# Which expert block uses the third buffer for its second weight matrix, in a fused attention, MLP and expert kernel

## The reference

```python
x = attention(q, k, v)                   # window of 64 keys, 4 x 576 tokens, 8 heads of 64
h = x @ w_in                             # 2304 x 512 times 512 x 2048
x = (h * tanh(softplus(h))) @ w_out      # 2048 x 512
do_compute = x @ w_skip > 0              # other tokens leave as they are
e_idx = argmax(x @ w_gate)               # one of 8 experts
for e in range(8):
    h = maximum(x[mask] @ w1[e], 0)      # w1: 512 x 1024
    y[mask] = gate_w * (h @ w2[e])       # w2: 1024 x 512
out = x + y
```

## Time and profile before

| | |
|---|---|
| three runs | 710.62, 712.65, 714.82 us (median 712.65) |
| the profiled execution | 713.13 us, of it span 711.5 us |
| TensorE (PE) busy | 682.2 us (96%), 4958 matmuls |
| VectorE, ScalarE, GpSimd busy | 488.1, 357.4, 254.2 us |
| mean granted TensorE clock | 0.989 |
| expert blocks | 12, the last 11 from 552.1 us on |

### The profile page before, as it was taken

One profiled execution on the slowest core, in us unless ns is written; L12 is line 12 of the kernel. 1 busy time (PEld: TensorE's weight loads), 2 busy tenths in 40 slices (PEclk: granted clock), 3 DMA queues, 4 the chain that ended last, 5 costly groups with the idle time before them and its releaser, 6 DMA issues. The chain is left out here.

```text
span 711.5 us, 13645 instructions
## 1 busy us (share of the span) xinstructions
PE 682.2 (96%) x4958; PEld 604.0 (85%) x4958; DVE 488.1 (69%) x940; ACT 357.4 (50%) x784; POOL 254.2 (36%) x231
## 2 busy tenths in 40 slices
PE   6898999999999999999999999999999979999995
PEld 5776898879898989888989888987988969899894
DVE  5797767867776885785786686679589545455352
ACT  5555566555554565456545555453554053443350
POOL 4312342443352343353344344335553331221221
PEclk9899999999999999999999999999999999999998
DMA  9734131151244132125115114102647799999940
GB/s 275 236 101 141 46 98 38 38 98 44 69 91 104 50 78 82 39 63 109 38 38 134 39 37 99 38 1 60 237 140 262 228 392 354 346 345 357 342 176 2
DMA packets 62835, 97.16 MB, mean 137 GB/s; under 512 B 23015, under 2 KB 27111, under 8 KB 62769
## 3 DMA queue, kind: packets, MB, share of 16 engines
q1 hardware_dynamic: 59152, 91.01, 42.0%
q0 software_dynamic: 3168, 4.51, 2.1%
q10 hardware_dynamic: 448, 0.79, 0.4%
HBM read 84.97 MB, written 13.73 MB: 139 GB/s over the span
## 5 line engine op out<-in xcount | busy, mean ns | idle before, releaser
L1552 POOL TENSOR_TENSOR q_sb<-n_sb,r_sb 128x512 f32<-128x512 f32 x72 | 94.3, 1309 | 287.1 <-DVE a_sb L1141 163.0
L628 PE MATMUL Y<-wout_hi,g_hi 128*128 128x512 f32 x272 | 111.6, 410 | 3.2 <-ACT g_hi L885 3.0
L609 PE MATMUL H<-x_hi,win_hi 128*128 128x256 f32 x384 | 112.4, 293 | 2.0 <-DVE x_lo L1075 1.9
L609 PE MATMUL H<-x_hi,win_lo 128*128 128x256 f32 x384 | 108.9, 284 | 0.0
L609 PE MATMUL H<-x_lo,win_hi 128*128 128x256 f32 x384 | 108.8, 283 | 0.0
L628 PE MATMUL Y<-wout_lo,g_hi 128*128 128x512 f32 x272 | 107.3, 395 | 0.0
L1558 POOL TENSOR_TENSOR g_lo<-g_sb,g_hi 128x512 fp32r<-128x512 f32 x68 | 88.2, 1297 | 2.5 <-ACT g_hi L885 1.9
L721 PEld LDWEIGHTS H<-xT,w 128*128 128x128 f32 x768 | 87.6, 192 | 1.0
L721 PE MATMUL H<-xT,w 128*128 128x128 f32 x768 | 88.0, 275 | 0.0
L1121 DVE TENSOR_SCALAR u_sb<-e_sb 128x512 f32<-128x512 f32 x72 | 34.0, 472 | 73.8 <-ACT e_sb L870 73.0
L885 ACT CAST g_hi<-g_sb 128x512 fp32r<-128x512 f32 x68 | 42.2, 620 | 74.6 <-DVE g_sb L1154 72.4
(11 more groups left out here) (205 smaller groups left out, 1408.0 us busy)
## 6 DMA issues: line engine op xcount, KB each, us to landing
w<-moe_w SPq DMA_DIRECT2D x23, 2048.0 KB, 10.9
kT<-k_T SPq DMA_DIRECT2D x32, 256.0 KB, 3.0
vw<-v_w SPq DMA_DIRECT2D x32, 256.0 KB, 3.0
y_rows<-ytile SPq DMA_DIRECT2D x36, 128.2 KB
out_rows<-ytile SPq DMA_DIRECT2D x36, 128.0 KB
win<-moe_w_in SPq DMA_DIRECT2D x8, 512.0 KB, 8.5
qbd<-q_T SPq DMA_DIRECT2D x64, 64.0 KB, 2.6
wout<-moe_w_out SPq DMA_DIRECT2D x8, 512.0 KB, 7.9
```

The lines of the kernel that those rows point to most:

```text
L609: last = nc.tensor.matmul(HM3[J % 3][:, f, :], wt[:, j, d, f * P:(f + 1) * P], xt[:, c % 2, d, :], start=(n == 0), stop=(n == 3 * DB - 1))
L628: last = nc.tensor.matmul(Y[t][:, :], gt[:, J % 2, lo:lo + P], wt[:, 2 * j + f, :], start=(j == 0 and f == 0 and wt is wout_hi and gt is g ...
L1552: nc.gpsimd.tensor_tensor(q_sb[:, :], n_sb[:, J % 2, :], r_sb[:, J % 2, :], ALU.mult).then_inc(q_ok, 1)
```

## The change

Three things change.

- `w2t` holds the `w2` of block 3 (`spare(b)`: b is `EARLY`, which is 3) in place of block 2's. It is allocated ahead of `ot`, so that it shares memory with slices 0 to 3 of `wout_hi`. SP loads it in the last chunk, right behind block 1's `w1`, once slice 3 of the last chunk is multiplied down. Block 2's `w2` goes into buffer 0, when block 0's `expert_down` is done and block 2's rows are gathered. The load of block 3's `w2` after block 1 is gone.
- Block 3's expert is fixed with the second pick: `lowest_left` now has six dependent steps and runs in tick 0 of the last chunk; `pick_third` leaves that expert out as well.
- GpSimd waits for the placed tokens of chunk c - 2 in tick 1 of chunk c, in place of those of c - 1 in tick 7. For chunk 7's tokens the wait stays in tick 7 of the last chunk.

```diff
             with ExitStack() as raw:
                 w2 = sb("w2", [P, 2, EFB * D], FP32, raw)
             w2_lo = sb("w2_lo", [P, 2, EFB * D], F32R, exp_)
+            with ExitStack() as raw:
+                w2t = sb("w2t", [P, EFB * D], FP32, raw)
+            w2t_lo = sb("w2t_lo", [P, EFB * D], F32R, exp_)
             ot = sb("ot", [P, 2, D], FP32, exp_)
...
-        LSTEPS = 4
+        LSTEPS = 6
...
-        def third(b):
-            return isinstance(b, int) and b == 2
+        def spare(b):
+            return isinstance(b, int) and b == EARLY
...
         def w2_there(eng, b, bh, slot_):
-            if third(b):
+            if spare(b):
                 eng.wait_ge(w2t_in, 16)
-            elif slot_ % 2 == 0 and not (isinstance(b, int) and b == 0):
-                eng.wait_ge(w2_in[0], loaded(bh, slot_) - 16)
+            elif slot_ % 2 == 1 and not (isinstance(b, int) and b == 1):
+                eng.wait_ge(w2_in[1], loaded(bh, slot_) - 16)
...
                     sp.wait_ge(g1_ok, NJ * NC)
                     load_w2(es[1], 1)
                     load_w1(es[1], 1)
+                    sp.wait_ge(lowest, LSTEPS)
+                    e4 = early_expert(EARLY)
+                    sp.wait_ge(g2_ok, NJ * c + 4)
+                    load_w2t(e4)
                 if c > 0:
                     store_rows(c - 1)
...
             store_rows(NC - 1)
-            sp.wait_ge(g2_ok, NJ * NC)
+            sp.wait_ge(bz_ok, 1)
             sp.wait_ge(xs_in[2], 16)
-            load_w2t(e3)
-            sp.wait_ge(lowest, LSTEPS)
-            e4 = early_expert(EARLY)
+            load_w2(e3, 0)
             sp.wait_ge(bh_ok, 4)
             load_w1(e4, 1)
-            sp.wait_ge(bz_ok, 2)
-            load_w2(e4, 1)
             sp.wait_ge(tstep, TSTEPS)
...
             def pick_second():
...
+                lowest_left()
...
                 step, count = steps(lowest, 0)
-                atmax = df[:, 1, :]
-                step(nc.vector.tensor_tensor(atmax, early[:, :], rev[:, 0, :], ALU.mult))
+                shut, atmax = first[:, 0, :], df[:, 1, :]
+                step(nc.vector.tensor_scalar(shut, early[:, :], -1.0, 1.0, ALU.mult, ALU.add))
+                step(nc.vector.tensor_tensor(atmax, shut, rev[:, 0, :], ALU.mult))
                 step(nc.vector.reduce_max(turn[:, 0:1], atmax, AX.X))
+                step(nc.vector.scalar_tensor_tensor(out=shut, in0=rev[:, 0, :], scalar=turn[:, 0:1], in1=early[:, :],
+                                                    op0=ALU.is_equal, op1=ALU.add))
...
             nc.vector.tensor_copy(q_sb[:, :], PTB[:, :]).then_inc(yT1_ok, 1)
-            lowest_left()
             rest_of_w2(1, 1, 2)
...
                 if c > 0 and j == 6:
                     scatter_tokens(c - 1)
-                if c > 0 and j == 7:
+                if c > 1 and j == 1:
+                    all_placed(c - 2)
+                if c == NC - 1 and j == 7:
                     all_placed(c - 1)
```

More of the change, by code:

```diff
@@ L185, in build @@
             cbi_i = sb("cbi_i", [P, NV], I32, exp_)
-            with ExitStack() as raw:
-                w2t = sb("w2t", [P, EFB * D], FP32, raw)
-            w2t_lo = sb("w2t_lo", [P, EFB * D], F32R, exp_)
         with ExitStack() as exp_:
@@ L328, in blocks @@
                         block_of(i * RING + n, i, n)
-        def third(b):
-            return isinstance(b, int) and b == 2
+        def spare(b):
+            return isinstance(b, int) and b == EARLY
         def w2_raw(b, slot_):
-            return w2t[:, :] if third(b) else w2[:, slot_ % 2, :]
+            return w2t[:, :] if spare(b) else w2[:, slot_ % 2, :]
         def w2_rest(b, slot_):
-            return w2t_lo[:, :] if third(b) else w2_lo[:, slot_ % 2, :]
+            return w2t_lo[:, :] if spare(b) else w2_lo[:, slot_ % 2, :]
         def w2_there(eng, b, bh, slot_):
-            if third(b):
+            if spare(b):
                 eng.wait_ge(w2t_in, 16)
-            elif slot_ % 2 == 0 and not (isinstance(b, int) and b == 0):
-                eng.wait_ge(w2_in[0], loaded(bh, slot_) - 16)
+            elif slot_ % 2 == 1 and not (isinstance(b, int) and b == 1):
+                eng.wait_ge(w2_in[1], loaded(bh, slot_) - 16)
             else:
@@ L804, in expert_block @@
                     expert_up(b, bh, slot_, half)
-                mid = EFB // 2 if third(b) else 0
+                mid = EFB // 2 if isinstance(b, int) and b == 2 else 0
                 if mid:
@@ L1258, in pick_third @@
                 step(nc.vector.tensor_tensor(now, nextrow[:, :], ecap[:, :], ALU.subtract))
-                step(nc.vector.scalar_tensor_tensor(out=held, in0=early[:, :], scalar=-float(BIG), in1=now,
+                step(nc.vector.scalar_tensor_tensor(out=held, in0=first[:, 0, :], scalar=-float(BIG), in1=now,
                                                     op0=ALU.mult, op1=ALU.add))
```

## The result

| | before | after |
|---|---|---|
| median of 20 runs each | 711.70 us | 714.27 us |
| lowest and highest | 708.97 to 714.82 | 712.18 to 716.69 |
| ratio after to before | | 1.0041, 95% interval 1.0027 to 1.0054 |
| the profiled execution | 713.13, span 711.5 | 712.60, span 711.0 |

The change makes the kernel 2.6 us slower. The forecast summed its terms to +0.1, at 712.8; measured are +2.6. (The medians differ by 2.6. Of that, 2.3 us are in the first 70 us, which the change doesn't touch (the same transposes start at 67.97 and at 65.71). So what follows compares intervals inside a profile, and uses further profiles of both kinds.

What follows compares the result with a forecast made beforehand. The prediction took TensorE to set the time. Its terms, -1.3 + 0.9 + 0.5 + 0 = +0.1 us, gave 713.2 on the profiled execution, forecast as 712.8 against the median of 712.65, with a range of 709.5 to 717.0.

Steps and rivals of the forecast that it cites:

- GpSimd's wait in tick 1: Chunk 1: without the scatter wait in tick 7, TensorE's 1.31 us wait for `g_lo` goes: -1.3, bounds -1.3 and 0.
- The pick in tick 0: Last chunk: six VectorE steps ahead of `g_hi` make TensorE wait +0.9 us near 500, bounds 0 and +1.1.
- the rival's mechanism: Last chunk's pick: a GpSimd operation holds one of VectorE's new steps, adding 2.6 us, 715.4; chance 0.03.
- Block 2's `w2`: Load issued at 559.4 as before, arriving no sooner without block 3's load behind it: 0, bound -1.5; stall of 3.92 us stays.
- The faster rival: Block 2's matrix comes sooner without block 3's load, and its stall could go: -5.7, 707.0; chance 0.13.
- The load in the last chunk: `w2t` loaded behind block 1's matrices: 2.1 MB, 5.2 us of all DMA engines, cost 0 on SP's queues.
- GpSimd's small DMAs under that load: Chunk 7's scatter +2.6 us, block 2's gather -1.6; middle taken, +0.5, counted in full.
- the prediction's own sign of being wrong: TensorE waits before block 2's rows' transpose, rows land after 561, or block 2's stall differs by over 1 us.
- The half that was to come back: Block 2's gather, once SP's transfers are over, takes at most 3.1 us against 4.7: -1.6.
- The slower rival: The third load pushes block 2's rows back by the whole 5.2 us: +4.8, 717.5; chance 0.19.
- the clock behind the stall: Behind block 2's stall TensorE runs 2.8 us at 1.2 GHz, losing about 1.4 us; said to stay.
- The bounds: Whole kernel: the terms' bounds add up to -3.5 (-1.3 + 0.9 - 1.6 - 1.5) and +3.7 (0 + 1.1 + 2.6).

Runs made afterwards that it cites:

- e1: The kernel before with only GpSimd's wait for chunk c - 2's tokens moved to tick 1 (last chunk keeps tick 7): 710.25 us, ratio 0.9973.
- e3: The changed kernel with GpSimd's wait put back into tick 7 of every chunk: 715.13 us, ratio 1.0045.
- e2: The kernel before with only the fourth expert's pick moved to tick 0 of the last chunk, in six steps: 711.92 us, ratio 1.0003.
- e11: e7 with gathers issued ahead of the wait for output rows, and the fourth expert's six steps in tick 2 of the last chunk: 708.48 us, ratio 0.9929.
- e4: The changed kernel again, unaltered, for a second profile and more runs: 714.49 us, ratio 1.0034.
- e5: The changed kernel with the load of block 3's `w2` moved ahead of block 1's matrices, near 517: 711.63 us, ratio 0.9976.
- e7: The changed kernel with e5's edit and without SP's wait for block 2's rows ahead of block 2's `w2`: 712.63 us, ratio 0.9987.
- e8: e1's kernel without SP's wait for block 2's rows, so `w2t` is issued near 552: 710.94 us, ratio 0.9967.

## Why the prediction was right or wrong

**GpSimd's wait in tick 1: right.** Forecast -1.3; the wait of 1.31 is gone, and e1 alone gives -1.9 with an interval from about -3.6 to -0.1. The size was read from one execution: the waits of 0.6 and 0.2 us in e3 and e2 make the mean of three profiles 0.7.

**The pick in tick 0: right.** Forecast a wait of 0.9 for `g_hi` near 500; it is 0.79 at 498. In tick 0 GpSimd held none of the steps, as the order of operations had it; e11 shows that the rival's mechanism is real one tick further on.

**Block 2's `w2`: right.** Its time from issue to cast is 10.6 us against 10.8, and over the seven profiles 10.1 to 11.3 (after, e3, e4, e5) against 10.7 to 11.7 (before, e1, e2); block 3's load behind it had not held it up. Block 3's first cast waits for no DMA. The faster rival fails with it: the load wasn't slow because of what was removed.

**The load in the last chunk: right in its place, wrong in its size.** The prediction's term for "GpSimd's small DMAs under that load" is the one that was mis-sized. It put +0.5, the middle between -1.6 and +2.6. The seven profiles give +2.7, just above the upper bound, and the prediction's own sign of being wrong came: TensorE waits before the transpose of block 2's rows. In the means, 1.0 of the 2.7 fall between the scatter and the load of token numbers, for which the term had up to +2.6. The load of token numbers, which it put at nothing, takes 1.6 more up to the gather. The half that was to come back, a quicker gather once SP's transfers are over, didn't: from the gather's issue to that of block 2's `w2` are 5.1 to 5.6 us with the load (558.98 - 553.72 in e4) and 4.6 to 5.9 without, 0.2 more in the mean and not 1.6 less. The row taken for it, block 1's gather in an otherwise quiet stretch, resembled nothing behind block 2's token numbers, where `w1` and the output rows are moved in both kernels. The slower rival had the mechanism with half its price: 2.7 us fall on the line of rows 7 where it put 5.2. That the idle engines took up the rest, as the prediction argued against it, fits but isn't shown. The routed rows of chunk 7 were put near 547 and landed at 548.95, which is 551.6 in the time of the profile before; that cost nothing.

**Missed: the clock behind the stall.** The forecast kept 2.8 us of slow clock. The two profiles of the changed kernel have 6.0 and 4.9, for stalls of 3.8 and 4.0; e1, with a stall of 2.3, has none. e3 has 3.4 us of it behind its wait for the rows. The lines of e4 and e1:

```profile
576.20:581.10 4.90, 4.85 (x12) 3.82 (x13) 0.50 (x1) 0.00 (x0) 1.14 (x2) 0.50 0.90 367
```

```profile
572.90:575.70 2.80, 2.78 (x12) 2.31 (x13) 0.47 (x1) 0.00 (x0) 0.00 (x0) 1.00 1.05 402
```

The first is e4's, the second e1's, both over the first half of block 2's `expert_down`. The other runs suggest that these profiles happened to be slow for long. The mean granted clock of the whole kernel is 0.985 in both, and 0.9876 over the 32 runs of the changed kernel beside 0.9880 over the 35 of the kernel before on e4's chip. That is 0.3 us of slow clock more for the change, uncertain by about 1 us either way. It covers the whole kernel, so the stretch behind the stall isn't told by it alone.

**The sum again**, with the terms of the profiles: -1.3 + 0.8 + 2.7 = +2.2 against +2.6 measured. The 2.7 is TensorE's, from block 1's transpose to block 4's, and has the slow clock in it. Two terms are uncertain by about 1 us: the first is -0.7 by the mean of three profiles, and the clock's share of 1.2 in the 2.7 is larger than all the runs together have. That the sum comes so near is in part luck.

**The bounds.** The lower one, -3.5, was summed with +0.9 for the pick, whose own lower bound is 0; it should have been -4.4. The measured +2.6 is inside either way, but the range of 709.5 to 717.0 holds the base of 712.65 too, and so left the direction open.

**The base.** The median of three runs, 712.65, stood 0.95 above that of twenty; the 1.5 between 712.8 and 714.27 looks small by luck, for the change itself was missed by 2.5.

## What to carry to other kernels

Idle DMA engines aren't free if a line of small dependent transfers runs through them: here 2 MB in the gap before it delayed the end of a line of a scatter, a load of 512 bytes and a gather by 2.7 us. Put an early load where no such line is waiting (e5), and look at which one transfer the next large load waits for before moving a load that nobody waits for. When a stall is removed, follow the in-order queue that comes next: e7 won block 2's stall and lost it at block 4, until the gather no longer stood behind a wait it didn't need.

## What the runs showed of the hardware

- Small DMAs under large ones: the load of 512 bytes of token numbers took from 6.0 to 9.6 us from its issue to the instruction that needs it, with transfers of SP in flight, in all thirteen profiles. With 2 MB more in flight the last of the scatter's packets started 4.4 to 4.6 us after its issue, without them 1.2 to 2.9. The Trainium skill ("DMA: Bandwidth & Descriptors", section "Queues, rings and completion order") says that each engine goes round robin between queues; no run here shows the order inside an engine, but a delay of 2.7 us by a load of some 5.2 us (an estimate, from the rate in rows 11) is less than standing behind all of it.
- An operation of VectorE on 128x8 elements took 2.79 us in rows 13 and 1.26 in e11, each until GpSimd's operation ended. In the profile before, a reduction over 128x8 took its 0.15 us at 493.73 while GpSimd's `q_sb` ran from 493.26 to 494.53, and the operation behind it, at 493.92, took 0.63, until 494.55. The Trainium skill ("SBUF — State Buffer", section "Who interferes with whom") says the same of operations with two inputs in SBUF and of some with one, and excepts reductions; these rows agree.
- A stall of TensorE of 3.8 to 4.0 us was followed by 2.8, 4.9 and 6.0 us of work at 1.2 GHz in three profiles. Of three waits of 2.1 to 2.3 us, those of e3 (before block 2's transpose) and e8 (before block 4's) were followed by 3.4 us and that of e1 by none. Waits of nearly equal length thus cost 1 us or more apart.
